# Loading the second group of early weights behind chunk 22's rows, in a kernel of attention and two MLPs

## The reference

```
state = gamma * state + k_t (outer) v_t          # per head, 4 x 8 heads, 768 steps, head size 64
y_t   = q_t @ state / sqrt(64)
x     = y as 3072 tokens x 512
x     = relu(x @ w_in)**2 @ w_out                # 512 -> 2048 -> 512
xn    = x / rms(x) * g
out   = (silu(xn @ w_gate) * (xn @ w_val)) @ w_out2   # 512 -> 1536 -> 512
```

## Time and profile before

| | |
|---|---|
| median of 3 runs | 1062.05 us |
| the profiled execution's own time | 1062.24 us |
| its span, first to last instruction | 1060.5 us |
| TensorE busy | 1050.8 us (99%) |
| VectorE busy | 882.0 us (83%) |
| ScalarE busy | 609.2 us (57%) |
| GpSimd busy | 331.8 us (31%) |
| granted TensorE clock | 1.00 throughout |

### The profile page before, as it was taken

The page is one execution under the profiler, slowest core; times in us unless marked ns, Lnnn a source line. Parts: engine busy times, 40 slices in busy tenths (PEclk is TensorE's granted clock), DMA queues, the critical chain, the costliest instruction groups (busy, mean ns, idle before and its releaser), DMA issues.

```text
span 1060.5 us, 15146 instructions
## 1 busy us (share of the span) xinstructions
PE 1050.8 (99%) x5742; PEld 870.1 (82%) x5742; DVE 882.0 (83%) x935; ACT 609.2 (57%) x879; POOL 331.8 (31%) x244
## 2 busy tenths in 40 slices
PE   8989999999999999999999999999999999999999
PEld 6878888888888888888888888888888888888887
DVE  5887989879779878789899988978886986978696
ACT  4875765557664666654674645556445555544453
POOL 1864550005530015430034554005444102544000
DMA  9999568654438644365642335632225751140456
GB/s 365 414 419 417 206 230 267 214 191 139 179 126 273 216 144 156 139 258 195 221 146 96 119 120 219 217 120 81 60 65 154 261 194 60 46 117 21 138 192 186
DMA packets 82759, 195.74 MB, mean 185 GB/s; under 512 B 30584, under 2 KB 39416, under 8 KB 75648
## 3 DMA queue, kind: packets, MB, share of 16 engines
q1 hardware_dynamic: 76960, 189.74, 51.4%
q10 hardware_dynamic: 5728, 5.04, 1.4%
HBM read 152.17 MB, written 42.48 MB: 184 GB/s over the span
## 4 chain that ended last, share of the span: by engine, by line
PE 96%; DMA 3%; SPq 0%; issue 0%; ACT 0%
PE Y L898 13%; PE Y L900 13%; PE Y L899 13%; PE X L898 9%; PE Z L898 9%; PE Z L900 9%; PE X L899 9%; PE Z L899 9%; PE X L900 9%; DMA qkv_sb<-qkv 3%; PE Z L849 1%; PE X L820 1%; PE Y L820 1%; PE R L873 1%; PE Z L839 1%; PE R L849 0%
## 5 line engine op out<-in xcount | busy, mean ns | idle before, releaser
L743 POOL TENSOR_TENSOR w_ops<-raw_w,w_ops 128x512 fp32r<-128x512 f32 x90 | 127.9, 1421 | 497.1 <-ACT w_ops L1027 497.0
L1091 ACT CAST ops<-hid 128x1024 fp32r<-128x1024 f32 x147 | 154.6, 1054 | 155.6 <-PE Y L900 53.3
L1492 DVE TENSOR_TENSOR ops<-hid,ops 128x1024 fp32r<-128x1024 f32 x147 | 179.9, 1226 | 37.9 <-ACT ops L1091 37.4
L743 POOL TENSOR_TENSOR w_ops<-sums_w,w_ops 128x512 fp32r<-128x512 f32 x120 | 167.4, 1398 | 120.9 <-ACT w_ops L1027 120.3
L898 PE MATMUL Y<-ops,w_ops 128*128 128x512 f32 x360 | 140.1, 389 | 0.0
L900 PE MATMUL Y<-ops,w_ops 128*128 128x512 f32 x360 | 140.1, 389 | 0.0
L899 PE MATMUL Y<-ops,w_ops 128*128 128x512 f32 x360 | 140.1, 389 | 0.0
L1116 ACT ACTIVATE gt<-gt 128x512 f32<-128x512 f32 x72 | 45.1, 633 | 111.7 <-DVE gt L1712 38.9
L898 PE MATMUL Y<-ops 128*128 128x512 f32 (+1 forms) x264 | 100.3, 380 | 0.0
L899 PE MATMUL Y<-ops 128*128 128x512 f32 (+1 forms) x264 | 100.1, 379 | 0.0
L900 PE MATMUL Y<-ops 128*128 128x512 f32 (+1 forms) x264 | 100.1, 379 | 0.0
(11 more groups left out here) (182 smaller groups left out, 2249.4 us busy)
## 6 DMA issues: line engine op xcount, KB each, us to landing
ops<-item_scratch SPq DMA_DIRECT2D x147, 512.0 KB, 3.4
raw_w<-w_f SPq DMA_DIRECT2D x30, 1024.0 KB, 5.2
qkv_sb<-qkv SPq DMA_DIRECT2D x17, 1024.0 KB, 9.6
item_scratch<-hid SPq DMA_DIRECT2D x30, 512.0 KB, 3.3
y_scratch<-hid SPq DMA_DIRECT2D x12, 512.0 KB, 5.8
raw<-y_scratch SPq DMA_DIRECT2D x3, 2048.0 KB, 9.6
raw<-w_b SPq DMA_DIRECT2D x5, 1024.0 KB, 4.9
out<-hid SPq DMA_DIRECT2D x36, 128.0 KB, 5.3
```

Of the source, the lines that this page charges most:

```text
L743: nc.gpsimd.tensor_tensor(w_ops[:, k, 1], front_w_source(m, k), f32(w_ops[:, k, 0]), ALU.subtract).then_inc(w_lo, 1)
L1091: nc.scalar.copy(hop_at(bk, n)[:, 0], hid[:, 2 * g:2 * g + 2, OPERAND[k], :])\
L1492: nc.vector.tensor_tensor(hop[:, 1], hid[:, 2 * g:2 * g + 2, OPERAND[k], :], f32(hop[:, 0]), ALU.subtract).then_inc(own_lo if bk.own_place ...
```

## The change

The second group is loaded at one point, behind the load of chunk 22 (n = 17, when chunk 17 is done), and no longer in halves behind the loads of chunks 16 and 17 (n = 11 and 12). All eleven GpSimd steps of the first group come first and then all of the second; the casts of the second group move to chunks 20, 21 and 22, and the last of them (item 13) into `first_run`, between `high_front(0, 3)` and `save_p5(0)`. In `first_run` `save_p5(0)` moves ahead of `high_front(0, 4)`, and `high_w(1, 0)` behind `high_front(0, 5)`. SP stores item 0 right behind item 6. The held stores of chunks 18 to 22 are issued in ScalarE's turn for chunk 23, and no longer in that for chunk 22.

```diff
--- before.py
+++ after.py
@@ -404,22 +404,20 @@
         def tokens(ps):
             return ps[:].rearrange("p z n -> p (z n)").rearrange("p (t d) -> p t d", t=4)
 
-        EARLY = [(0, u) for u in range(9)] + [(1, 0), (1, 1), (0, 9), (0, 10)] + [(1, u) for u in range(2, 11)]
+        EARLY = [(quad, u) for quad in range(2) for u in range(11)]
 
         def early_at(x):
-            return 10 + x * 14 // 22
+            return 10 + x * 14 // 22 if x < 11 else 21 + (x - 11) // 4
 
         def early_casts(n):
 
             at, found = 0, []
-            for x, (quad, u) in enumerate(EARLY):
+            for x, (quad, u) in enumerate(EARLY[:11]):
                 if unit_item(u) is not None:
                     at = max(at, early_at(x) - (2 if ITEMS[unit_item(u)] in SUMMED else 3))
-                    if 7 * quad + unit_item(u) >= EARLY_PLACES - 2:
-                        at = max(at, NCH - RING + 1)
                     if at == n:
                         found.append((quad, unit_item(u)))
-            return found
+            return found + [(1, i) for i, late in enumerate((20, 21, 21, 21, 22, 22)) if late == n]
 
         def unit_item(unit):
             return (None, None, 0, 1, None, 2, 3, 4, None, 5, 6)[unit]
@@ -516,14 +514,15 @@
                     load_early_quad(0, (n - 4) // 2)
                 if n == 8:
                     sp.dma_start(gains[:], rms_g).then_inc(consts_loaded, 16)
-                if n in (11, 12):
+                if n == NCH - RING - 2:
                     sp.wait_ge(w_lo, 7)
-                    load_early_quad(1, n - 11)
+                    load_early_quad(1, 0)
+                    load_early_quad(1, 1)
             for i in (4, 5):
                 store_item(0, i)
             sp.wait_ge(quad_lo, 7)
             load_raw_w(1)
-            for i in (6, 7, 8, 9, 10, 11, 0, 1, 2, 3, 12, 13):
+            for i in (6, 0, 7, 8, 9, 10, 11, 1, 2, 3, 12, 13):
                 store_item(*divmod(i, 7))
 
             def load_items(bk, lo, hi):
@@ -1169,11 +1168,12 @@
 
                 seed(0)
                 high_front(0, 3)
+                high_quad(1, 6)
+                save_p5(0)
                 high_front(0, 4)
-                save_p5(0)
                 save_u2(0)
+                high_front(0, 5)
                 high_w(1, 0)
-                high_front(0, 5)
                 high_front(0, 6)
                 act.wait_ge(*done(0, 3))
                 nc.scalar.activation(hid[:, 0:2, A, :], X[:], ACT.Relu).then_inc(relu_x, 1)
@@ -1341,11 +1341,9 @@
                     high_front(0, (4, 13, 19).index(n))
                 if n < HELD:
                     store_x(n)
-                elif n == NCH - 2:
-                    for held in range(HELD, NCH - 1):
+                elif n == NCH - 1:
+                    for held in range(HELD, NCH):
                         store_x(held)
-                elif n == NCH - 1:
-                    store_x(n)
             for t in range(TILES):
                 bk = BackRun(t, False)
                 for p in range(R1):
```

## The result

The changed kernel takes 1065.52 us (median of 8 runs, 1064.55 to 1067.13) where the kernel before, run beside it, takes 1062.18 us (8 runs, 1061.86 to 1063.52): ratio 1.003, 95% interval 1.002 to 1.0041, so 3.3 us slower. The forecast was 1060.8 us, in a range from 1059.3 to 1063.2. The profiled execution took 1065.43 us, with a span of 1063.7.

What follows compares the result with a forecast made beforehand. TensorE was taken as the bound, busy 1050.8 of 1060.5 us, with DMA waits for chunk rows to win. Attention's 1.84 us less 0.55 before step 6 gave 1.3 us: forecast 1060.8 us, range 1059.3 to 1063.2.

Steps and rivals of the forecast that it cites:

- Attention: Scores of chunks 18 to 21 lose 2.52 us of waits, chunk 23 waits 0.68 anew: attention ends 1.84 us earlier.
- The byte count: At 0.415 MB per us, the 1 MB load ahead of chunk 18's rows costs 2.53 us; chunk 23 gains nothing.
- step 6's cast: In run 0 it waits for item 11's store, taken to land at 95.0 us, between 94.4 and 95.5.
- that rival: Item 11's store still takes 16.7 us and lands at 103.5; step 6 begins at 108.2: 1069.3 us, chance 7%.
- bound of 94.0: Earliest useful landing of item 11's store: issue at 86.8 plus the 7.2 us of chunk 15 in the full queue.
- The step that failed: VectorE's low parts in run 0 end at 89.8, 92.9 and 94.9, wanted at 90.94, 93.66 and 96.38.
- without a neighbour: Step 6's low part on VectorE takes 1.21 us with no GpSimd operation beside it, ending at 97.3.
- a sign of being wrong: The prediction called itself wrong if, among other signs, steps 4 or 5 of run 0 wait for low parts.
- its sum's two terms: 1.84 us won in attention less 0.55 us of new wait before step 6 of run 0: 1.3 us.
- 0.45 us on GpSimd: Extra time for a GpSimd step meeting a two-input SBUF VectorE operation, counted twice before item 11's low part.
- the second rival: GpSimd holds up VectorE: step 3's low part and the combination lose 1.1 us each; 1062.1 us, chance 20%.
- The held stores: Issued on ScalarE from about 83.2 to 86.4 us, costing nothing while the seed before step 2 keeps 0.8 us cover.

Runs made afterwards that it cites:

- experiment 5: Changed kernel with item 0 stored behind items 6 to 11 again: 1065.56 us, ratio 1.0026 to the kernel before.
- the last version of experiment 8: Changed kernel, second group's last five GpSimd steps on VectorE, run 1's weight subtractions held behind run 0's low parts: 1062.3 us, ratio 0.9999 to the kernel before.
- experiments 1: Changed kernel with GpSimd's last three second-group steps on 16 of 512 columns, output incomplete: 1062.49 us, ratio 1.0006 to the kernel before.
- experiment 2: Changed kernel with run 1's weight subtractions on GpSimd held until run 0's seven low parts are done: 1063.24 us, ratio 1.0009 to the kernel before.
- experiments 1 and 3: The latter: changed kernel, GpSimd's last three second-group steps on 16 columns and run 1's weight subtractions held behind run 0's low parts: 1062.29 us, ratio 0.9997.
- the last version of 7: Changed kernel, step 3's cast in chunk 22's turn, run 1's weight subtractions behind run 0's low parts, item 0's store and item 13's cast later: 1063.77 us, 1.0004.
- second profile of the changed kernel: Changed kernel run once more, unedited, on another chip with another profile: 1065.67 us, ratio 1.0026 to the kernel before.
- experiment 7, first version: Changed kernel with step 3's cast moved ahead into ScalarE's turn for chunk 22: 1064.48 us, ratio 1.002 to the kernel before.
- experiment 4: Kernel before, with six needless GpSimd subtractions added in run 0 and no load, store or cast moved: 1067.82 us, ratio 1.0054.
- the moved cast in 6: Changed kernel with item 13's cast behind step 4's cast in ScalarE's queue: 1066.1 us, ratio 1.0024 to the kernel before.

## Why the prediction was wrong

- **Attention: right.** Chunk 23 was issued at 67.5 and landed 10.5 us later, at 78.0 (predicted 77.8); new wait 0.87 us (0.68); end 1.65 us earlier (1.84). The byte count held for the rows.
- **GpSimd and ScalarE: right within about half a microsecond.** First sum 76.22 (75.9), item 11's low part done at 87.26 (86.8, where the prediction's own terms add up to 86.7), `seed` ends at 87.92 (87.4) without TensorE waiting, step 6's cast waits for the store until 94.66 (95.0). The five stores of items 7 to 11 took 5.9 to 7.3 us from issue to landing, not 17: the forecast's sign was wrong, but not by that rival. That the store landed where it was forecast is in part luck. The 95.0 came from the bytes in the queue, item 0's among them, and those changed little (experiment 5); the landing followed from the issue at 87.3 and the 7.3 us behind it, which is nearer to the bound of 94.0 that the prediction had worked out from the earlier trace rows.
- **The step that failed** is "VectorE's low parts then end at 89.8, 92.9 and 94.9 [...] covered by 1.1, 0.8 and 1.5 us", and behind it the 1.21 us "without a neighbour" for step 6. They ended at 91.03, 94.40 and about 99.6, and TensorE waited for steps 4 and 5, which the prediction had named as a sign of being wrong. Of its sum's two terms the first measured 1.65 us for 1.84; in place of the second, 0.55, run 0 lost 4.9 (step 6 at 104.18, where 100.94 less 1.65 is 99.29). The ledger up to the addition's end (104.13, before 100.60): it starts 0.62 us earlier (88.92 for 89.54), then loses 0.9 on step 3's low part, 1.1 on the combination, 1.1 on the first sum and 1.7 on the last two low parts (4.52 for 2.84), and wins the 0.5 us for which it stood before step 5 in the earlier trace rows. That makes 3.7 us, where 3.5 were measured. Before, those operations were:

```profile
89.54 1.23 DVE L1404 TENSOR_TENSOR ops<-raw,ops 128x1024 fp32r<-128x1024 f32 x1 [4.24 <-ACT ops L1046]
90.68 1.22 DVE L1446 TENSOR_TENSOR raw<-raw 128x1024 f32<-128x1024 f32 x1
...
92.95 0.69 DVE L1538 TENSOR_TENSOR sums_w<-raw_w 128x512 f32<-128x512 f32 x1
```

  I had charged 0.45 us on GpSimd for meetings in attention. On VectorE in run 0 there was only what the 1.42 us of the earlier trace rows hold of a meeting, 0.2 us over 1.21 for each of three low parts, and nothing for the combination and the sums. Apart from meetings, the 94.9 also left out the three half-width sums that VectorE does between the low parts of steps 4 and 5, though the second rival has them. In the last version of experiment 8, without a meeting, step 5's low part ended 3.0 us behind step 4's (93.21 and 96.2): from 92.9 that gives 95.9 (an estimate), a cover of 0.5 us and not 1.5. The stretch had much less room than the prediction saw.
- **The second rival named the mechanism and sized it too low.** It let two operations lose 1.1 us each, beside the last three steps of the second group, and left out run 1's weight subtractions. Those begin as soon as ScalarE has cast, whether VectorE is behind or not: once it is 2 us late they meet three more of its operations. So it came out at 1062.1 in place of 1065.5. That is also why experiments 1 and 2 each win back over 2 us of 3: with either half gone VectorE is near enough to its time.
- **The held stores.** Their edit changes no order: ScalarE has no cast in chunk 23's turn, so that the stores stood behind the same instructions in both. They were later because of the casts ahead of them. In the changed kernel step 2 didn't wait for `seed`, but with 0.5 us of cover (87.92 and 88.42) where 0.8 were counted; in experiments 1 and 3 and the last version of 7 it waited 0.2 to 0.4 us.
- **A term the prediction lacked, worth little.** Within step 5, after 2.23 us without work, TensorE's granted clock fell to its lower level, 1.2 GHz (0.50), as the windows of the changed kernel show:

```profile
100.00:102.00 2.00, 2.00 (x8) 1.58 (x8) 2.00 (x2) 0.00 (x0) 2.00 (x2) 0.75 0.99 410
102.00:104.00 2.00, 2.00 (x6) 1.17 (x4) 2.00 (x2) 0.00 (x0) 2.00 (x2) 0.50 0.70 209
```

(columns: PE, PEld, DVE, ACT, POOL busy, clock, DMA share, GB/s). Step 5 took 4.40 us instead of 2.72. But step 6 begins 0.05 us behind the end of VectorE's addition, at 104.13, and not behind step 5's own end: the slow clock lay in a wait, and cost only the 0.24 us of a longer step 6 (2.96 for 2.72). In the second profile of the changed kernel, and in experiments 4, 5 and 6, step 6 also begins within 0.1 us behind that addition.

The Trainium skill (SBUF — State Buffer, "SBUF: two separate sides") says that a VectorE operation with two SBUF inputs and a GpSimd operation that reads SBUF take one port pair as an exclusive lock for a whole instruction. The trace agrees: each long operation of VectorE is longer by 0.9 to 1.1 us, less than one GpSimd step of 1.27, and those with an input in PSUM (L1686 and L1690, 1.21) are not longer beside a busy GpSimd.

## What to carry to other kernels

Before moving work of GpSimd in time, list which VectorE operations with two SBUF inputs it will then run beside, and charge each of them with most of a GpSimd step, not the average of a few rows. Follow the second turn too: work that is released by a third engine doesn't wait for the one that fell behind, and meets more of it. A gain at a DMA-bound place is only kept if the stretch into which the deferred work falls has room on its tightest chain, here 0.34 us at step 6. And a wait that keeps one engine off another's way has its own price further on: look for it behind the stretch that it mends, here 0.4 us and more in run 1.

## What was not expected of the hardware

TensorE's granted clock stayed at 2.4 GHz through idle times of 1.18 and 1.44 us in run 0 (experiment 7, first version) and of 2.09 us in attention (experiment 2), and went to 1.2 GHz after those of 2.23 to 3.29 us, in all five profiles that had one: the two of the changed kernel, and those of experiment 4, experiment 5 and the moved cast in 6. No run varied an idle time by itself, so these are rows and no rule.
